# Loads, sums and copies in another order, and filling products at three waits of TensorE, in a fused attention, mixture-of-experts and Mish kernel

## The reference

```python
# 1. attention: q, k, v are (2, 8, 576, 64); factor 4
q_d = q.reshape(B, H, 144, 4, D).mean(axis=3)      # k_d, v_d the same
out_d = softmax(scale * q_d @ k_d.T) @ v_d         # pooled attention
out_up = np.repeat(out_d, 4, axis=2)
mask = np.abs(pos[:, None] - pos[None, :]) < 4     # seven keys around a query
out_local = softmax(where(mask, scale * q @ k.T, -1e9)) @ v
x = (out_up + out_local)                           # to (1152, 512)
# 2. mixture of experts, top 1 of 8, at most 288 tokens an expert
expert_idx = argmax(x @ w_gate); gate_w = softmax(x @ w_gate)[expert_idx]
y = relu(x_of_expert @ w1[e]) @ w2[e]              # 512 -> 1024 -> 512
x = gate_w * y                                     # back at each token's place
# 3. dense layer
h = x @ w_in                                       # 512 -> 2048
out = (h * tanh(softplus(h))) @ w_out              # 2048 -> 512
```

## Time and profile before

| | |
|---|---|
| median of 3 runs | 476.28 us (473.52, 476.28, 480.75) |
| the profiled execution | 477.65 us |
| its span, first to last instruction | 475.5 us |
| TensorE products busy, share of the span | 447.9 us, 94% |
| chain of work that ended last, share on TensorE | 84% |
| attention | 0 to about 100 us |
| experts | about 105 to 263 us |
| dense layer | from there to the end |

### The profile page before, as it was taken

The page is one execution under the profiler, slowest core; times in us unless marked ns, Lnnn a source line. Parts: engine busy times, 40 slices in busy tenths (PEclk is TensorE's granted clock), DMA queues, the critical chain, the costliest instruction groups (busy, mean ns, idle before and its releaser), DMA issues.

```text
span 475.5 us, 10038 instructions
## 1 busy us (share of the span) xinstructions
PE 447.9 (94%) x3380; PEld 412.8 (87%) x3381; DVE 280.7 (59%) x665; ACT 230.1 (48%) x631; POOL 137.2 (29%) x136
## 2 busy tenths in 40 slices
PE   8869898989879999999999999999999999999993
PEld 7658687878879999999999898899988999988982
DVE  7879577679202102102111599888888888888873
ACT  2756665642313323332223566655665655656541
POOL 9587325111000000000004455433253333433202
PEclk9979899599989999999999999999999999999998
DMA  9999999232867988996846234123141121321001
GB/s 186 196 193 152 166 379 347 101 112 74 293 240 243 357 300 281 350 311 207 281 159 207 82 88 45 43 88 90 44 143 57 49 83 45 90 110 44 1 0 66
DMA packets 72143, 74.97 MB, mean 158 GB/s; under 512 B 32816, under 2 KB 47920, under 8 KB 72112
## 3 DMA queue, kind: packets, MB, share of 16 engines
q1 hardware_dynamic: 70384, 69.84, 51.0%
q0 software_dynamic: 1728, 4.72, 2.6%
HBM read 65.11 MB, written 9.44 MB: 157 GB/s over the span
## 4 chain that ended last, share of the span: by engine, by line
PE 84%; DVE 6%; ACT 4%; issue 3%; DMA 1%; SPq 1%; POOLq 0%; POOL 0%; ACTq 0%; DVEq 0%
PE ps L1174 79%; ACT pr L703 2%; PE ps L1256 2%; PE ps L1421 1%; DMA qk_tok<-in_q 1%; PE ps L1302 1%; SPq L431 1%; DVE mx L928 1%; DVE sme L935 1%; PE ps L1251 0%; DVE qT L901 0%; ACT prT L686 0%; DVE kdT L887 0%; DVE qdT L887 0%; DVE gL L1080 0%
## 5 line engine op out<-in xcount | busy, mean ns | idle before, releaser
L637 POOL TENSOR_TENSOR wiL<-raw,wiH 128x512 fp32r<-128x512 f32 x48 | 62.5, 1303 | 251.5 <-ACT wiH L686 148.3
L1174 PE MATMUL ps<-xe,raw 128*128 128x128 f32 (+2 forms) x512 | 71.7, 302 | 4.7 <-issue 3.9
L1174 PEld LDWEIGHTS ps<-xe,raw 128*128 128x128 f32 x512 | 70.4, 194 | 5.6 <-issue 4.4
L1174 PE MATMUL ps<-hid,raw 128*128 128x128 f32 (+2 forms) x512 | 70.8, 297 | 0.0
L1174 PEld LDWEIGHTS ps<-hid,raw 128*128 128x128 f32 x512 | 69.0, 191 | 0.0
L1174 PE MATMUL ps<-x2H,wiH 128*128 128x384 f32 x192 | 65.1, 339 | 0.3 <-DVE x2L L1080 0.3
L1174 PE MATMUL ps<-x2L,wiH 128*128 128x384 f32 x192 | 65.3, 340 | 0.0
L1174 PE MATMUL ps<-x2H,wiL 128*128 128x384 f32 x192 | 64.6, 337 | 0.0
L1174 PE MATMUL ps<-woH,gH 128*128 (+1 forms) x144 | 56.9, 395 | 2.5 <-DVE gL L1080 2.5
L1174 PE MATMUL ps<-woH,gL 128*128 (+1 forms) x144 | 57.2, 397 | 0.0
L1174 PE MATMUL ps<-woL,gH 128*128 (+1 forms) x144 | 56.7, 394 | 0.0
(11 more groups left out here) (140 smaller groups left out, 769.1 us busy)
## 6 DMA issues: line engine op xcount, KB each, us to landing
raw<-in_moe_w SPq DMA_DIRECT2D x32, 1024.0 KB
raw<-in_moe_w_in SPq DMA_DIRECT2D x24, 512.0 KB
x_by_expert<-x_sb SPq DMA_DIRECT2D x1, 4608.0 KB, 15.5
xg<-x_by_expert SPq DMA_DIRECT2D x8, 512.0 KB, 3.6
wo_in<-in_moe_w_out SPq DMA_DIRECT2D x8, 512.0 KB
v<-in_v SPq DMA_DIRECT2D x4, 576.0 KB
qk_tok<-in_k SPq DMA_DIRECT2D x8, 256.0 KB, 4.8
qk_tok<-in_q SPq DMA_DIRECT2D x8, 256.0 KB, 5.1
```

The lines of the kernel that those rows point to most:

```text
L637: nc.gpsimd.tensor_tensor(wiL[:, r, :, :], raw_wi_tile(r), wiH[:, r, :, :].bitcast(F32), ALU.subtract).then_inc(s_wil, 1)
L1174: return T.matmul(out_, a, b, start=start, stop=stop, skip_group_check=True)
```

## The change

It has four parts.

1. **Fills.** Sixteen filling products are added at each of three places of TensorE's list: in `probs_t(2)` behind the wait for the PSUM copy and ahead of the wait for the normed probabilities (round 3); in round 4 ahead of the wait for the pooled q and k; and in round 8 behind the scores and ahead of the first product of that round. Each is a loop of four turns with four products.
2. **Shorter loops.** The 50 fills at the start go in ten turns of 5, not five of 10; the 16 ahead of a pooled tile in four turns of 4, not two of 8. Their numbers stay.
3. **GpSimd.** The last V sum (j = 3) moves behind the copies of the first two pooled tiles.
4. **SyncE.** x(e) is loaded behind unit 0 of expert e and ahead of unit 1, in the iteration of e, and no longer one iteration ahead, behind unit 2. Unit 2 waits for the whole result of expert e-1, and no longer for its first half. The last expert is an iteration of the loop.

```diff
-TURN_LOADS, TURN_DOWN, TURN_LOCAL = 10, 8, 6
+TURN_LOADS, TURN_DOWN, TURN_LOCAL, TURN_WAIT = 5, 4, 6, 4
+WARM_SUMS, WARM_NORM, WARM_PROBS = 16, 16, 16
...
             sp.wait_ge(s_xg, 16)
-            sp.wait_ge(s_xet, K1)
-            sp.wait_ge(s_xt3, 1)
-            load_x(1)
-
-            def expert(e, last):
+
+            def expert(e):
 
                 sp.wait_ge(s_h, e * M1 - M1 // 2)
                 load_unit(e, 0)
+                sp.wait_ge(s_xet, e * K1)
+                sp.wait_ge(s_xt3, e)
+                load_x(e)
                 sp.wait_ge(s_h, e * M1)
                 load_unit(e, 1)
-                sp.wait_ge(s_w2u, e)
+                sp.wait_ge(s_y, e * M2)
                 load_unit(e, 2)
-                if not last:
-                    sp.wait_ge(s_xet, (e + 1) * K1)
-                    sp.wait_ge(s_xt3, e + 1)
-                    load_x(e + 1)
                 sp.wait_ge(s_h, e * M1 + 1)
                 load_unit(e, 3)
                 load_wo(e)
 
-            with sp.Fori(1, E - 1) as e:
-                expert(e, False)
-            expert(E - 1, True)
+            with sp.Fori(1, E) as e:
+                expert(e)
...
-            for j in range(KH, B * KH):
-                sum_v(j)
+            sum_v(KH)
+            pool.wait_ge(s_vd, KH + 1)
+            place_od(FIRST_DOWN[0])
+            place_od(FIRST_DOWN[0] + 1)
+            sum_v(KH + 1)
             pool.wait_ge(s_vd, B * KH)
-            for n in range(NS):
+            for n in range(FIRST_DOWN[0] + 2, NS):
                 if is_down(n):
                     place_od(n)
...
             def probs_t(n):
                 down = STEPS[n][0] == "down"
+                if n >= 1:
+                    pe.wait_ge(s_ptc, n)
+                if n == HELD - 2:
+                    keep_warm_in_turns(6, WARM_NORM, TURN_WAIT)
...
-                if n >= 1:
-                    pe.wait_ge(s_ptc, n)
...
                         pe.wait_ge(s_exp, n - 1)
+                    if n == FIRST_DOWN[0]:
+                        keep_warm_in_turns(2 * (n % 2), WARM_SUMS, TURN_WAIT)
                     if n in FIRST_DOWN:
                         pe.wait_ge(s_qd, HELD + 1 if n == FIRST_DOWN[0] else NT)
...
                     counts(n)
+                if n == local_step(HELD) + 1:
+                    pe.wait_ge(s_kTc, NT)
+                    keep_warm_in_turns(TB, WARM_PROBS, TURN_WAIT)
                 for m in attended(n):
```

## The result

The changed kernel took 488.4 us (median of 4 runs, 484.78 to 492.29), and the kernel before, run beside it, 475.1 us. The ratio is 1.0266, with a 95% interval from 1.0171 to 1.0361: slower, by 13.3 us in the medians. The ratio is taken from means without the slowest execution of each kernel (492.29 and 480.75), so it is a little under 488.4 / 475.1 = 1.028. The forecast was 481.5, and 488.4 lies at the very edge of its range of 471.0 to 488.5.

What follows compares the result with a forecast made beforehand. TensorE, 94% busy, was taken as the bound, with half clock behind its waits and DMA close in the experts. Attention -2.0, late x +6.5, clock fall +1.7, fetch wait -1.0: +5.2 on 476.3 gives 481.5 us, range 471 to 488.5.

Steps and rivals of the forecast that it cites:

- rival 2: Whole kernel: every new wait drops the clock, waits at their upper bound, fetch unchanged; +13.2, 489.5 us; chance 0.20.
- x too late: Experts: x queued behind other loads makes TensorE wait, 2.4 us each in experts 2 and 4; +6.5 us in all.
- the landing at 13.1 us: Experts: x(e+1) lands 13.1 us after the hidden layer begins, wanted at 10.7 (128 columns) or 13.1 (160).
- The slower case of the prediction's own range: Experts 2 to 4: at 349 GB/s x lands at 14.4 us, with waits of 3.7, 1.3 and 3.7.
- Expert 0: Expert 0: unit 0 goes ahead of x(1), which lands at 125.2 or later against 124.9; +0.3 to +0.8 us.
- Clock falls behind the waits: Experts: one fall to half clock behind the two new waits for x; +1.7 us, between 0 and +5.
- The wait of 3.63 us: At 129.56 us: TensorE's next-pass code arrives late, perhaps slowed by SyncE's loads, and an emptier queue helps; -1.0 us.
- a sign of being wrong: Signs against the forecast: half clock near 30 us, no gap at the turns of x, or the 3.63 us wait gone.
- The attention, -2.0: Attention: fills hold the clock, round 5 ends 2.5 us earlier, V windows cap that at 1.3; -2.0 us, -2.6 to -1.3.
- Shorter loops, 0: Fill loops: four turns of 4 follow without gaps like two of 8; 0, between 0 and +0.3 us per loop.
- GpSimd's order, 0: Attention: GpSimd's copies aren't last in either order, so its new order gives between 0 and 0.2 us by itself.
- 83 to 97 us, 0: Half-clock stretch behind small gaps, not aimed at by the change; 0, though its going would give back about 4 us.

Runs made afterwards that it cites:

- experiment 11: The changed kernel with 16 fills ahead of each of TensorE's waits for x; 486.93 us, ratio 1.0322 to the kernel before.
- before_again: The kernel before, unchanged, run once more for a second profile; 473.88 us.
- x_early: The changed kernel with x loaded one expert ahead again, unit 2 still waiting for the whole result; ratio 0.9998 to the kernel before.
- v_nofills: The kernel before with the first batch's V windows loaded earlier and GpSimd's first two copies ahead of its last two sums, no fills added; 470.13 us, ratio 0.9995.
- experiments 3 to 5: The changed kernel with, one at a time: unit 2 on the first half again (1.0110), x ahead of unit 0 (1.0038), x an expert ahead again (0.9998).
- rest_only: The changed kernel with SyncE's old load order, keeping fills, shorter loops and GpSimd's order; 469.63 us, ratio 0.9984 to the kernel before.
- v_first: rest_only with the first batch's V windows loaded ahead of the second's V rows and GpSimd's last two sums behind the first two copies; 471.13 us, ratio 0.9915.
- sp_only: The kernel before with only the new order of SyncE's loads; 487.84 us, ratio 1.0342 to the kernel before.
- v_tail: v_first with 16 more fills in the last two rounds of the attention; 467.59 us, ratio 0.9934 to the kernel before.
- u2_early: The changed kernel with unit 2 waiting for the first half of the result again, x in its new place; ratio 1.0110 to the kernel before.

## Why the prediction was right or wrong, point by point

The direction, and the place and cause of the loss, were right; its size was taken too small: +13.3 us where the forecast had +5.2. The result lies outside the forecast's own band of 477 to 486 us and in the tail above 485.8 that had a chance of 0.22. That it is inside the range at all is luck of 0.1 us. Its number is nearer to rival 2 (489.5 us), but not all of rival 2 came: the waits went beyond its upper bound (12.7 against 9.5), the clock fell behind two of five, and the old wait shrank where that rival had it unchanged.

- **x too late: right in mechanism, under-sized.** Forecast 6.5 us, measured 12.7, beyond the upper end of 9.5. The step that failed is the landing at 13.1 us behind the start of the hidden layer. In expert 2 it is 161.7 - 147.0 = 14.7, and in experts 1 and 3 it is 14.2 and 15.1. The loads in the window 149 to 162 us of the changed kernel, and the rate (last figure) between the first byte and the landing:

```profile
DMA packets 2395, 4.71 MB, mean 362 GB/s; under 512 B 96, under 2 KB 96, under 8 KB 2395
...
xg<-x_by_expert SPq DMA_DIRECT2D x1, 512.0 KB, 9.5
xg<-x_by_expert SPq DMA_DIRECT2D x1, 64.0 KB, 9.4
```

```profile
149.40:161.60 12.20, 8.50 (x77) 8.31 (x75) 1.22 (x1) 3.08 (x9) 0.00 (x0) 1.00 1.02 372
```

  The rate was 372 GB/s, not 392 (+0.6 us on 4.19 MB). I had left out x's second load, of 64 KB, for which TensorE waits too (+0.2 us). And the 12.2 us at 372 GB/s moved 4.54 MB, 0.28 MB more than three units, w_out and both loads of x, 4.26 MB: by this sum, packets of the next unit, issued at 154.5, moved ahead of x's last ones (+0.8). Whose packets they were the trace doesn't say. The start, 2.4 us behind the hidden layer's, was as forecast. So 10.7 becomes 12.2. For 128 columns the wait is then 14.7 - 10.9 = 3.8, as the rows show, and the same delay opens a wait of 1.8 us in expert 3 and of 0.9 in expert 1, which I had at 0 and not at all. This was the error: a landing at exactly the time of need (13.1 against 13.1 for 160 columns) was counted as no wait, though anything later costs in every such expert. The slower case of the prediction's own range, 349 GB/s with a landing at 14.4 us and waits of 3.7, 1.3 and 3.7, was close in experts 2 to 4; expert 1 was missing from it too, and I had chosen near the other end.
- **Expert 0.** Forecast 0.3 to 0.8 us, measured 2.35. x(1) was issued 5.8 us behind the start of the hidden layer (114.70 against 108.86) and landed 7.5 us later, while I took 5.1 from before and 6.3.
- **Clock falls behind the waits.** Forecast one of 1.7 us, measured two of 1.7. The price of a fall was right, the number of them followed the longer waits. That the waits cause them is borne out by all traces together (experiment 11). The 1.43 us that rival 2 leaned on was no such sign: the fall behind it isn't in `before_again`, and no wait for x of up to 1.82 us brought one.
- **The wait of 3.63 us.** Forecast -1.0, for a fetch slowed by SyncE's queue. The cause was wrong: `x_early` and `v_nofills` show the wait with 177 and 393 GB/s alike. 3.0 us of it went and, by the sums in experiments 3 to 5, because TensorE had stood at x(1) for 2.35 us just before. The Trainium skill, DMA: Bandwidth & Descriptors, section Queues, rings and completion order, says that a DMA engine takes its queue rows in turn, a packet at a time; by that rule a fetch is hardly held up by SyncE's loads, and these runs agree with it (2.40 us of wait at 393 GB/s, 2.99 at 177). The prediction had named this wait's end as a sign of being wrong; it went almost (0.64 us) and the loads were late all the same, so it was no sign of that. In the account of the experts above it is a gain of 3.0 us of wait and 1.7 of clock, but one that the wait for x(1) has paid for with 2.35.
- **The attention, -2.0.** `rest_only` measures -0.8, between -3.2 and +1.7, with the other two parts in it. The steps were right: both loops lie in waits for VectorE, round 5's scores start 2.6 us earlier (37.12 before, 34.50 after), and the V windows stop the gain at 51.0 us (forecast 51.4). `v_first` and `v_nofills` show both sides of that cap. But that the clock then stays up was wrong: it fell at other places, a different one in most kernels. And the 1.3 us to be won from the fall at 52.7 weren't there to win in every execution, since `before_again` hasn't that fall.
- **Shorter loops, 0.** The row behind a set of 16 in four turns of 4 starts 1.20 us after it (33.30 to 34.50), as with two turns of 8.
- **GpSimd's order, 0.** Its copies end at 47.6, well ahead of 51.0. It wasn't tried alone.
- **83 to 97 us, 0.** Right that the change doesn't touch it, but `before_again` shows that the stretch isn't a property of the kernel.

By the medians the sum is -0.8 for the rest and, for SyncE's order, 14 (13.3 + 0.8) to 16 (`sp_only`), where the forecast had -2.0 and +7.2. The account of the trace has 11.4 of that; the rest isn't placed.

## What to carry to other kernels

A load that is moved behind others in the same queue is late by the bytes ahead of it, and a wait added to one of those others is paid by it too: work out the landing against the need for every iteration, count each load and its small companion, and treat "just in time" as late. When a gap is filled, look at once for what is late next, because here neither the fills nor the earlier V windows gave anything alone, and together they gave 0.7 to 0.9%. One profiled execution can hold a long stretch of half clock that the next one doesn't have, so take it twice before giving it a cause.

## What the runs showed of the hardware that I had not expected

- The place of the half clock wanders from kernel to kernel and from execution to execution, at the same work: 84 to 96 us has a granted clock of 0.50 in one execution of the kernel before and 0.90 in another. With the early gaps filled, the changed kernel has it at 81 to 83 and 98 to 104 us, and one execution of `v_tail` has none from 10 us on. Executions of one kernel differ along with it: by 3.2 us for 0.01 of the mean granted clock.
- In the experts the clock falls only behind a wait. Of the waits for x, it fell behind five of five of 2.83 us and more, behind three of six from 1.87 to 2.52, and behind none of the nine from 0.55 to 1.82.
- The wait that TensorE has once, ahead of the hidden layer of expert 1 in the loop's second pass, is 2.3 to 3.6 us long, whether the queue moves 393 or 177 GB/s, and time that TensorE spends just before it, waiting for x(1) or in fills, is subtracted from it nearly in full.
- A queue that was empty moved 372 GB/s over the 12.2 us from its first byte to the landing of x, and 349 over 10.3 us in `u2_early`. The 392 that I had reckoned with is the better of two windows of before; the other has 349. By the bytes, packets of the unit behind moved ahead of the last ones of x.
